# Attention feeding a mixture of experts: two weight casts, one load and one GpSimd wait are moved in the attention's first part

## The reference

```python
scores = scale * np.matmul(q, k.transpose(0, 1, 3, 2))
psi_rel = np.log1p(np.abs(rel))                      # 576 x 576
psi_i = np.log1p(np.maximum(pos[:, None], 1.0))
h = np.maximum((psi_rel / psi_i)[..., None] @ w1 + b1, 0.0)   # 32 hidden
scores = scores + (h @ w2).transpose(2, 0, 1)[None]  # one bias matrix per head
attn = exp(scores - max) / (sum + 1e-9)
x = attn @ v                                         # to 1152 tokens x 512
```

```python
p = domain_probs / (domain_probs.sum(-1, keepdims=True) + 1e-9)
for e in range(4):
    out += p[:, e:e + 1] * (np.maximum(x @ w1[e], 0.0) @ w2[e])
```

## Time and profile before

| | |
|---|---|
| median of 3 runs | 602.77 us (601.95 to 602.98) |
| the profiled execution's own time | 602.77 us |
| its span, first to last instruction | 601.0 us |
| TensorE busy | 575.7 us, 96% |
| VectorE busy | 295.4 us, 49% |
| ScalarE busy | 263.3 us, 44% |
| GpSimd busy | 119.8 us, 20% |
| share of the chain that ended last | PE 85%, DVE 4%, ACT 3%, issue 2%, DMA 2% |

### The profile page before, as it was taken

One profiled execution on the slowest core, in us unless ns is written; L12 is line 12 of the kernel. 1 busy time (PEld: TensorE's weight loads), 2 busy tenths in 40 slices (PEclk: granted clock), 3 DMA queues, 4 the chain that ended last, 5 costly groups with the idle time before them and its releaser, 6 DMA issues.

```text
span 601.0 us, 10144 instructions
## 1 busy us (share of the span) xinstructions
PE 575.7 (96%) x4024; PEld 470.9 (78%) x4024; DVE 295.4 (49%) x619; ACT 263.3 (44%) x522; POOL 119.8 (20%) x176
## 2 busy tenths in 40 slices
PE   3879999899999999999999999999999999999997
PEld 1357886566677888878888788998899899889986
DVE  7967775786356433662436433551263236135511
ACT  4767774775446434562446442450053025204400
POOL 5165886000001423133242311000000000000000
PEclk9889999899999999999999999999999999999999
DMA  4799941674474513662255203231142214121101
GB/s 149 245 285 314 260 125 37 169 224 120 135 240 134 180 40 110 171 198 60 82 145 161 71 19 123 72 139 36 35 133 79 69 25 153 35 71 71 35 36 52
DMA packets 60655, 72.73 MB, mean 121 GB/s; under 512 B 23232, under 2 KB 39872, under 8 KB 60608
## 3 DMA queue, kind: packets, MB, share of 16 engines
q1 hardware_dynamic: 60416, 72.08, 39.1%
q10 hardware_dynamic: 192, 0.01, 0.0%
HBM read 59.10 MB, written 12.98 MB: 120 GB/s over the span
## 4 chain that ended last, share of the span: by engine, by line
PE 85%; DVE 4%; ACT 3%; issue 2%; DMA 2%; SPq 1%; POOL 1%; ACTq 0%; DVEq 0%; POOLq 0%
PE x_banks L1172 23%; PE x_banks L1155 19%; PE scores L1155 12%; PE scores L1172 10%; PE turn L1104 4%; PE scores L1135 4%; PE scores L1069 4%; PE x_banks L1135 2%; PE turn L1046 2%; PE scores L1046 2%; DVE hidden L752 2%; DMA v_more<-v_in 1%; ACT w_hi L961 1%; DVE w_lo L805 1%; POOL probs L695 1%
## 5 line engine op out<-in xcount | busy, mean ns | idle before, releaser
L695 POOL TENSOR_SCALAR probs<-probs,recip 128x576 f32<-128x576 f32 x72 | 54.0, 760 | 223.6 <-DVE recip L790 223.5
L805 DVE TENSOR_TENSOR w_lo<-w_raw,w_hi 128x1024 fp32r<-128x1024 f32 x64 | 79.6, 1243 | 21.3 <-ACT w_hi L961 21.3
L1155 PE MATMUL x_banks<-x_hi,w_hi 128*128 128x512 f32 (+2 forms) x232 | 82.5, 356 | 0.0
L1155 PE MATMUL x_banks<-x_hi,w_lo 128*128 128x512 f32 (+2 forms) x232 | 80.2, 346 | 0.0
L1155 PE MATMUL x_banks<-x_lo,w_hi 128*128 128x512 f32 (+2 forms) x232 | 80.1, 345 | 0.0
L946 ACT COPY probs_t<-turn 128x512 f32<-128x512 f32 (+2 forms) x88 | 43.7, 516 | 72.5 <-PE turn L1104 71.7
L775 DVE CUSTOM_DVE_ANT_0 probs<-scores,bias 128x576 f32<-128x576 f32 x72 | 52.0, 754 | 46.9 <-PE scores L1069 34.2
L1172 PE MATMUL x_banks<-w_hi,h_hi 128*128 128x512 f32 x184 | 74.4, 404 | 0.0
L968 ACT ACTIVATE h_hi<-x_banks 128x512 fp32r<-128x512 f32 (+2 forms) x58 | 27.7, 478 | 103.5 <-PE x_banks L1155 103.2
L1172 PE MATMUL x_banks<-w_hi,h_lo 128*128 128x512 f32 x184 | 71.9, 391 | 0.0
L1172 PE MATMUL x_banks<-w_lo,h_hi 128*128 128x512 f32 x184 | 71.9, 391 | 0.0
(11 more groups left out here) (123 smaller groups left out, 999.0 us busy)
## 6 DMA issues: line engine op xcount, KB each, us to landing
w_raw<-w_in SPq DMA_DIRECT2D x64, 512.0 KB, 3.5
qk_raw<-qk_t_in SPq DMA_DIRECT2D x16, 576.0 KB, 4.5
bias<-bias_scratch SPq DMA_DIRECT2D x16, 576.0 KB, 5.0
bias_scratch<-probs_t SPq DMA_DIRECT2D x18, 288.0 KB, 3.3
v<-v_in SPq DMA_DIRECT2D x24, 128.0 KB, 3.8
bias_scratch<-rows SPq DMA_DIRECT2D x8, 288.0 KB, 3.4
out_dram<-acc SPq DMA_DIRECT2D x8, 256.0 KB, 2.0
bias_scratch<-probs SPq DMA_DIRECT2D x5, 288.0 KB, 2.9
```

What stands on the lines that cost most here:

```text
L695: pool.tensor_scalar(tile, tile, recip[:, stat(f, p, j)], 1.0, ALU.mult, ALU.mult).then_inc(normed, 1)
L805: dve.tensor_tensor(lo, raw, hi.bitcast(F32), ALU.subtract).then_inc(w_lo_out, 1)
L1155: mm = pe.matmul(m_bank(n)[:, 0:width], w, x, start=k == 0 and part == 0, stop=k == MT - 1 and part == 2)
```

## The change

Four edits, all in the first 100 us of the program:

1. The chunks 0 and 1 are cast in the steps 10 and 12, no longer 4 and 15, and VectorE makes the low part in the same step as ScalarE makes the high part, no longer one step later.
2. Chunk 0 is loaded behind `load_bias0(3, 0)`, six calls later in SyncE's list.
3. GpSimd no longer waits for VectorE's 48 bias instructions before it splits pair 2.

```diff
-CHUNK_AT0 = (4, 15)
+CHUNK_AT0 = (10, 12)
...
                 rows_all_stored(EARLY)
                 load_bias0(0, 1)
                 load_bias0(1, 1)
-                load_chunk(0)
                 load_raw(4)
                 load_v(0, 2)
                 load_v(0, 3)
                 load_raw(5)
                 load_bias0(2, 0)
                 load_bias0(3, 0)
+                load_chunk(0)
                 load_bias0(2, 1)
...
                 for g in range(PLACES0):
-                    if g == 2:
-                        pool.wait_ge(hid_dve, ON_DVE * EARLY)
                     high_of_qk(g)
                     low_of_qk(g)
...
-                    if s - 1 in CHUNK_AT0:
-                        low_of_chunk(CHUNK_AT0.index(s - 1))
+                    if s in CHUNK_AT0:
+                        low_of_chunk(CHUNK_AT0.index(s))
```

## The result

The changed kernel is slower by 0.7%: 606.66 us median (605.56 to 607.79, four executions) against 602.36 us (601.79 to 602.98, four executions) for the kernel before, ratio 1.0072 with a 95% interval of 1.0044 to 1.0099. That is +4.3 us where the forecast was 608.9 us and +6.1. The profiled execution has a span of 604.7 us and its own time is 606.52 us.

What follows compares the result with a forecast made beforehand. The prediction took TensorE's stream to bound the kernel, early delays being carried to the end. GpSimd's removed wait +3.4, chunk 0's later load -0.5 and the moved casts +3.2 made +6.1 on 602.77: 608.9 us, range 605.0 to 611.5.

Runs made afterwards that it cites:

- v early: Kernel before, with v of pair 2 loaded together with v of pairs 0 and 1, ahead of SyncE's store wait: 602.57 us against 602.84, ratio 1.0000.

## What to carry to other kernels

A delay worked out at one engine has to be followed through the next waits until it meets TensorE at a place from which it is carried; each wait of a late engine for something else (here 1.89 us for a load) swallows up to its own length, less what the edit delays that something by, so look for such waits before adding. Where two chains lead to one place, here the score adds and v behind the stores in one list, an edit that delays both must be priced by the later of them, and one that relieves the second is worth nothing until the first is late too. Don't make an engine wait for another's result of the same step when a one-step-old one will do: here this cost 1.65 us for two casts, and a chunk's low part costs there in either order: one step later it makes GpSimd's `normalise` take 2.43 and not 1.47 us.

## What was not expected of the hardware

- The first GpSimd instruction of pair 3, on 128x576 values and issued amid VectorE's back-to-back bias instructions, took 0.68 to 1.03 us in four profiles and 9.55 and 9.96 us in two, with the same program in one pair of them. That of pair 2 got in in all seven profiles in which it was issued there (0.67 to 0.90 us). Which it is isn't told by when it starts (16.9 to 18.2 us after the stream's start in all, in no order). What decides it stays open. When the GpSimd instruction stands, VectorE isn't delayed by it; when it gets in, four bias instructions take 3.89 and not 1.73 us.
- The clock behind the same wait of 2.09 us of TensorE for block 18 is 1.2 GHz in nine profiles and 2.4 in five. TensorE's block 19, before and after:

```profile
115.82 2.10 PE L1046 MATMUL turn<-bias,w_block 128*32 128x288 f32 x16
```

```profile
121.16 1.18 PE L1044 MATMUL turn<-bias,w_block 128*32 128x288 f32 x16
```

  From that wait to the end of the span it is 486.1 to 486.5 us in the nine and 484.8 to 484.9 in the five, nothing between: such a stretch costs 1.2 to 1.7 us, and it isn't the edits that bring it. That is 0.2 to 0.3% of this kernel, as much as some of the effects here, and the reason for comparing stretches and medians, not single spans.
- No version here beats the kernel before: the best two, v early and edit 2 with chunk 0's cast in step 10, are at 1.0000 and 1.0002. Whether v early together with the later load of chunk 0 (which would remove the wait of ScalarE that took its place) gains something wasn't tried.
